# Three seams between the stages of a fused recurrence and two expert layers: rows, zero rows, weights and token blocks in another order

## The chip, the cores and the metric

The kernel runs on one core of a Trainium2 chip. The metric is the device time of one execution in microseconds (us); for the kernel before, it is the median of three runs.

## What is computed

A delta-rule attention feeds two mixture-of-experts layers. All arithmetic is in float32.

```python
# 4 batches x 8 heads, 768 tokens, head size 48
k_n = k / (norm(k) + 1e-6)
for t in range(S):
    y[t] = q[t] @ state
    state = state + beta[t] * outer(k_n[t], v[t] - k_n[t] @ state)
x = y as [3072 tokens, 384]
# first layer: 8 experts, F = 1024, one expert for each token (argmax of x @ w_gate)
out[mask] = gate_w[mask] * eom[mask, e] * (relu(x[mask] @ w1[e]) @ w2[e])
# second layer: 4 experts, F = 1024, every token in all of them
out += p[:, e] * (relu(x @ w1[e]) @ w2[e])
```

## The kernel before, in words

Five engines run their own written-out programs and meet at semaphores. A wait names a count; a DMA adds 16 when it has landed. There is no scheduler: the order in the source is the order on each engine.

**Attention.** The sequence is cut into NC = 12 chunks of 64 tokens. In chunk c TensorE does predict, solve, advance and read_out, and between them the products that prepare chunks c + 1 and c + 3 (level16, level32, gram, query) and the gate logits of chunk c - 1 (gates_turned L835, gates_product L844, gates_back). ScalarE (ACT) copies what they leave: gates_taken (L1168), left16_taken (L1150), values (L1145), x_taken (L1161), logits_turned, left32_taken (L1155). At the head of chunk 10 ACT calls first_expert_up (L1215 to L1218): it waits until the six pieces of w1 of expert 0 have landed, and casts them (the high part of a float32 that is split in two float32r parts). GpSimd (POOL) scatters the rows of each chunk by expert into the DRAM tensor x_rows (L583), whose 8 regions each end in up to 128 rows that tail_rows (L356 to L359) fills with zeros.

**Passes.** NPASS = 31 passes of 128 rows follow; each belongs to one expert, and every expert's last pass may be part zeros. SP loads the rows of pass s into the only buffer xs_in (L531) when pass s - 1 has taken its own. TensorE's `both(s)` is up(s) (18 matmuls), tokens_turned(s + 1) (3 transposes, L940), down(s - 1) (24 matmuls), hidden_turned(s) (8 transposes, L969). A product is three matmuls (high by high, high by low, low by high: L933 to L935). VectorE (DVE) does relus, turned, y_taken (L1688) and hidden (hTh L1680, hTl L1682). Weights of expert e + 1 are loaded and cast by ACT, and POOL makes their low part (L597). The keep_warm call (L929) multiplies ones 36 times between the attention and the first pass.

**Second layer.** The 3072 tokens are three blocks q = 0, 1, 2 of 8 tiles; 16 slices of 256 hidden units (v) each take three steps s, one for each block: up2 (33 matmuls in 7 sums, a scheme that forms [2x2] block products from sums of the operands), then down2 of the step before (8 tiles of 6 matmuls). The tokens of a block are first turned (turn(n), n = 8q + 0..7, 3 transposes, L997), copied by ACT (tokens_hi, L1306 to L1310), mixed by POOL (tokens_mixed, L646 to L652) and finished by DVE (tokens_lo L1751, mixed_lo L1756). Block 0 is turned during passes 22 to 25, blocks 1 and 2 at the end of the passes and inside the first steps. DVE also does summed (L1769), g_lo_taken (L1773), added (L1782) and once the gate values of all tokens (L1727 to L1744; shares_scaled is its second part, L1736 to L1744). The results leave by 24 indirect DMAs of POOL (L703), one for each tile.

The order on TensorE at the end of the passes is written out by hand:

```python
            up(NPASS - 1)
            down(NPASS - 2)
            hidden_turned(NPASS - 1)
            turn(QT)
            turn(QT + 1)
            down(NPASS - 1)
            turn(QT + 2)
            turn(QT + 3)
```

Here QT = 8. down(s) waits for hT_lo (DVE's hidden(s)) and for y_ok (DVE's y_taken(s - 2), which empties bank 4). turn(n) waits for x2T_read, which counts the tokens_lo that have emptied a bank.

## Time and profile before

| | us |
|---|---|
| median of 3 runs | 1475.72 (1472.4 to 1476.86) |
| the profiled execution, its own time | 1467.39 |
| its span, first to last instruction | 1465.5 |
| TensorE busy | 1393.4 (95%) |
| VectorE busy | 1030.3 (70%) |
| ScalarE busy | 344.8 (24%) |
| GpSimd busy | 375.8 (26%) |
| mean granted TensorE clock | 0.973 of full speed |

The 40 slices of the profile's page are 36.6 us each. TensorE is busy 9 tenths or more in nearly all slices from the fourth on; the exceptions are the slices at 293 to 366 us (8, 7), 366 to 403 us (8) and 659 to 696 us (7). In the same places the row of the granted clock leaves 9. The attention ends at about 350 us, the passes at about 664 us; the second layer takes the rest. The time of an execution is 1.9 us more than its span.

### The profile page before, as it was taken

How to read it: one execution, taken by the hardware profiler on the slowest of the kernel's cores; microseconds unless marked ns; L12 is line 12 of the kernel's file. 1: busy time of each engine (PE TensorE's matmuls, PEld its weight loads, DVE VectorE, ACT ScalarE, POOL GpSimd, SP SyncE). 2: the span in 40 equal slices, each digit the busy share in tenths (PEclk: the TensorE clock that was granted, in tenths of full speed). 3: DMA queues.
4: the chain of work that ended last, by engine and by line, in shares of the span. 5: the costliest groups of instructions: out<-in, count | busy, mean ns of one | idle time of the engine just before them, and what ended most of it. 6: DMA issues, size and time to landing. Idle time of an engine off the chain costs nothing.

```text
span 1465.5 us, 37247 instructions
## 1 busy us (share of the span) xinstructions
PE 1393.4 (95%) x14185; PEld 1277.8 (87%) x14186; DVE 1030.3 (70%) x1924; ACT 344.8 (24%) x810; POOL 375.8 (26%) x465
## 2 busy tenths in 40 slices
PE   5799999988899999997899999999999999999997
PEld 4789999977799999996899999999999999999996
DVE  5567777736566666667777777777777777777775
ACT  2345555431111111112211111111121111111111
POOL 1000101101444444337412121212212121212125
PEclk7999999989899999998999999999999999999999
DMA  6545554344433333010000000000000000000003
GB/s 132 112 98 105 126 107 116 83 121 141 142 108 109 109 109 109 18 39 22 11 12 21 11 21 11 22 11 21 11 22 20 12 21 11 21 11 21 11 11 119
DMA packets 101976, 85.67 MB, mean 58 GB/s; under 512 B 57520, under 2 KB 93488, under 8 KB 101872
## 3 DMA queue, kind: packets, MB, share of 16 engines
q1 hardware_dynamic: 83632, 49.32, 14.0%
q10 hardware_dynamic: 15168, 25.15, 5.3%
q0 software_dynamic: 3072, 9.71, 1.8%
q8 instruction: 77, 1.26, 0.4%
q14 instruction: 27, 0.22, 0.1%
HBM read 67.97 MB, written 16.18 MB: 57 GB/s over the span
## 4 chain that ended last, share of the span: by engine, by line
PE 89%; DMA 4%; DVE 3%; SPq 2%; issue 1%; ACT 1%; POOL 0%; ACTq 0%; POOLq 0%; DVEq 0%
PE bank L933 23%; PE bank L935 23%; PE bank L934 23%; PE bank L709 11%; PE bank L969 2%; PE bank L824 2%; PE bank L827 2%; PE bank L844 1%; ACT R L1123 1%; DMA kq_sb<-in_kq_dram 1%; PE bank L940 1%; SPq L449 1%; DMA inverse_blocks<-inverse 1%; DMA x_rows<-zeros 1%; PE bank L997 1%
## 5 line engine op out<-in xcount | busy, mean ns | idle before, releaser
L1784 DVE SCALAR_TENSOR_TENSOR y_all<-bank,aux_all,y_all 128x384 f32<-128x384 f32 x360 | 218.0, 616 | 102.3 <-PE bank L935 100.1
L1769 DVE TENSOR_TENSOR sums<-bank,sums 128x512 f32<-128x512 f32 x336 | 223.6, 688 | 60.0 <-PE bank L935 47.2
L933 PE MATMUL bank<-v2h,gTh 128*128 128x384 f32 x768 | 258.3, 336 | 3.0 <-DVE y_all L1782 2.3
L935 PE MATMUL bank<-v2h,gTl 128*128 128x384 f32 x768 | 257.7, 336 | 0.0
L934 PE MATMUL bank<-v2l,gTh 128*128 128x384 f32 x768 | 257.4, 335 | 0.0
L1322 ACT ACTIVATE gTh<-sums 128x512 fp32r<-128x512 f32 x192 | 110.9, 624 | 610.0 <-PE bank L935 608.0
L933 PEld LDWEIGHTS bank<-v2h,gTh 128*128 128x128 f32 x768 | 144.7, 188 | 5.8 <-DVE y_all L1782 2.7
L597 POOL TENSOR_TENSOR w_split_sb<-w_raw,w_split_sb 128x384 fp32r<-128x384 f32 (+1 forms) x98 | 107.0, 1142 | 165.6 <-ACT w_split_sb L1278 165.6
L934 PEld LDWEIGHTS bank<-v2l,gTh 128*128 128x128 f32 x768 | 144.7, 188 | 1.8
L1773 DVE SCALAR_TENSOR_TENSOR gTl<-sums,gTh 128x512 fp32r<-128x512 f32 x192 | 140.1, 770 | 7.3 <-ACT gTh L1322 4.3
L935 PEld LDWEIGHTS bank<-v2h,gTl 128*128 128x128 f32 x768 | 144.5, 188 | 0.0
L933 PE MATMUL bank<-w_split_sb,hTh 128*128 x248 | 86.5, 349 | 4.2 <-DVE hTl L1682 4.2
L682 POOL CAST v2h<-v_raw 128x384 fp32r<-128x384 f32 x32 | 15.3, 508 | 290.5 <-PE bank L935 290.5
L668 POOL CAST vA<-vA_raw 128x384 fp32r<-128x384 f32 (+1 forms) x48 | 24.3, 545 | 253.7 <-PE bank L935 253.6
L934 PE MATMUL bank<-w_split_sb,hTh 128*128 x248 | 84.1, 339 | 0.0
L935 PE MATMUL bank<-w_split_sb,hTl 128*128 x248 | 84.0, 339 | 0.0
L583 POOL DMA_INDIRECT x_rows<-rows_st,pos x24 | 26.3, 1097 | 215.9 <-PE bank L827 206.7
L933 PE MATMUL bank<-x_plain,vA 128*128 128x512 f32 x192 | 75.7, 394 | 6.2 <-DVE x_mixed L1756 6.2
L933 PE MATMUL bank<-w_split_sb,xsTh 128*128 (+1 forms) x186 | 76.9, 413 | 1.2 <-DVE xsTl L1664 1.2
L935 PE MATMUL bank<-x_plain,vA 128*128 128x512 f32 x192 | 76.4, 398 | 0.0
L934 PE MATMUL bank<-x_plain,vA 128*128 128x512 f32 x192 | 76.2, 397 | 0.0
L933 PE MATMUL bank<-x_mixed,vA 128*128 128x512 f32 x192 | 75.1, 391 | 0.0
(226 smaller groups left out, 2781.6 us busy)
## 6 DMA issues: line engine op xcount, KB each, us to landing
w_raw<-in_moe_w_dram ACTq DMA_DIRECT2D x14, 1536.0 KB, 7.1
xs_in<-x_rows SPq DMA_DIRECT2D x31, 203.0 KB, 2.4
v_raw<-in_moe_w_dram SPq DMA_DIRECT2D x15, 384.0 KB, 3.1
kq_sb<-in_kq_dram SPq DMA_DIRECT2D x28, 192.0 KB, 4.1
kt_sb<-in_kt_dram SPq DMA_DIRECT2D x24, 196.0 KB, 3.8
vt_sb<-in_vt_dram SPq DMA_DIRECT2D x24, 192.0 KB, 4.6
vA_raw<-in_moe_w_dram SPq DMA_DIRECT2D x15, 256.0 KB, 2.6
kq_sb<-in_kq_dram SPq DMA_DIRECT2D x14, 256.0 KB, 4.6
```

The costliest lines, as they stand in the source:

```text
L597: last = pool.tensor_tensor(lo[:, m, at_], raw[:, m, at_], hi[:, m, at_].bitcast(f32), ALU.subtract)
L709: return pe.matmul(dst, lhsT, rhs, start=True, stop=True)
L824: pe.matmul(bank[5 + p][half_rows(a), small(p, h)], kq_sb[half_rows(a), c % NKQ, 1, h], state[half_rows(a), c % 2, h], start=True, stop=False)
L827: last = pe.matmul(bank[5 + p][half_rows(a), small(p, h)], PT[half_rows(a), c % NPT, h], delta[half_rows(a), h], start=(c == 0), stop=True)
L933: pe.matmul(dst, lh, rh, start=first, stop=False)
L934: pe.matmul(dst, lh, rl, start=False, stop=False)
L935: return pe.matmul(dst, ll, rh, start=False, stop=last)
L969: ins = pe.transpose(bank[2 + half][:, 128 * m:128 * m + 128], h_sb[:, k0:k0 + 128], ident)
L1322: act.activation(sum_place(gTh, k), sums[:, SUM_TILE[k]], ACT.Relu).then_inc(g_hi, 1)
L1769: dve.tensor_tensor(out_, x, y, ALU.add).then_inc(sum_ok, 1)
L1773: dve.scalar_tensor_tensor(out=sum_place(gTl, k), in0=sums[:, SUM_TILE[k]], scalar=0.0, in1=sum_place(gTh, k).bitcast(f32), op0=ALU.max, o ...
L1784: dve.scalar_tensor_tensor(out=a, in0=src, scalar=share, in1=a, op0=ALU.mult, op1=ALU.add).then_inc(acc_ok, 1)
```

## The change

Seams one to three are the end of the attention, the first passes, and the way from the passes into the second layer; a fourth edit is at the end of the output.

1. **Weights of expert 0.** ACT's first_expert_up moves from the head of chunk 10 to behind values(11, 1) in that chunk.
2. **Rows and zero rows.** SP loads the rows of pass 1 (next_rows(1)) as soon as pass 0 has taken its own and the zero rows of expert 1 (second_zero) have landed, and only then issues the zero rows of experts 2, 4, 6. ACT issues the zero rows of expert 1 first, and those of 3, 5, 7 when the rows of pass 1 have landed (xs_load 32); its loads of the weights of expert 1 stand behind them. SP waits for all zero rows ahead of the rows of pass 2. Behind keep_warm 12 more products of ones, in float32r, are put.
3. **Last pass and token blocks.** The last pass has its own hTh_last, hTl_last, so that DVE's hidden(30) needn't wait for down(29). TensorE turns the first two tiles ahead of hidden_turned(30) and down(29), and spreads the other turns; down2(0) uses three banks, not two. On DVE hidden(30) comes first, y_taken(29) behind the first part of the gate values, shares_scaled behind four tokens_lo and a mixed_lo. The loads of vA and v2 and the cast of block 0's first tokens no longer wait for the last pass of expert 6; ACT does the cast of vA that POOL did. x_plain of blocks 0 and 1 change places in SBUF.
4. **Output.** POOL waits for two tiles at a time, but for the last two.

```diff
+        hTh_last = place("hTh_last", [128, KF, 128], f32r)
+        hTl_last = place("hTl_last", [128, KF, 128], f32r)
...
-        for q, (plain_at, mixed_at) in enumerate(((weights_base + 2 * w_size, weights_base),
-                                                  (common_end + 16384, weights_base + w_size),
+        for q, (plain_at, mixed_at) in enumerate(((common_end + 16384, weights_base),
+                                                  (weights_base + 2 * w_size, weights_base + w_size),
...
-            return bank[6 + n % 2 if n < 2 * QT else 3 + 2 * (n % 2) if n < 3 * QT - 2 else 5]
+            return bank[6 + n % 2 if n < 2 * QT else (3, 5, 0)[(n - 2 * QT) % 3]]
...
-               .then_inc(tail_zero if e else first_zero, 16)
+               .then_inc((first_zero, second_zero)[e] if e < 2 else tail_zero, 16)
...
+            sp.wait_ge(slots_ok, 1)
+            sp.wait_ge(second_zero, 16)
+
+            def next_rows(s):
+                sp.wait_ge(xsT_mm, s)
+                sp.wait_ge(aux_ok, s)
+                at_ = pass_i[0:1, 3, s:s + 1] if isinstance(s, int) else pass_i[0:1, 3, bass.ds(s, 1)]
+                row = sp.value_load(at_, min_val=0, max_val=NE * REG - 128)
+                load_rows(x_rows[bass.ds(row, 128), :])
+
+            next_rows(1)
             for e in range(2, NE, 2):
                 tail_rows(sp, e)
-            sp.wait_ge(slots_ok, 1)
-            sp.wait_ge(tail_zero, 16 * (NE - 1))
-            with sp.Fori(1, NPASS) as s:
-                sp.wait_ge(xsT_mm, s)
-                sp.wait_ge(aux_ok, s)
-                row = sp.value_load(pass_i[0:1, 3, bass.ds(s, 1)], min_val=0, max_val=NE * REG - 128)
-                load_rows(x_rows[bass.ds(row, 128), :])
+            sp.wait_ge(tail_zero, 16 * (NE - 2))
+            with sp.Fori(2, NPASS) as s:
+                next_rows(s)
...
+            up_weights_mixed(0)
             first_tokens()
-            up_weights(0)
             for j in range(BT):
                 tokens_mixed(j)
             down_weights(0)
             for j in range(BT, 2 * BT):
                 tokens_mixed(j)
             for v in range(1, NV):
-                up_weights(v)
+                up_weights_mixed(v)
+                up_weights_hi(v)
...
-                pool.wait_ge(acc_ok, QT * NQ * (NV - 1) + t + 1)
+                if t % 2 == 0 or t >= NT - 2:
+                    pool.wait_ge(acc_ok, QT * NQ * (NV - 1) + t + (2 if t < NT - 2 else 1))
...
+            for _ in range(12):
+                mul(bank[7][:, 0:128], ones_r[:], ones_r[:])
...
+                before = n - (1 if n < 2 * QT else 2)
                 if n >= 2:
-                    pe.wait_ge(x2T_read, n - 1)
+                    pe.wait_ge(x2T_read, before)
                 if n >= QT + 2:
-                    pe.wait_ge(x2T_raw, n - QT - 1)
+                    pe.wait_ge(x2T_raw, before - QT)
                 if n == 2 * QT:
                     pe.wait_ge(sum_ok, NSUM)
-                if n == 3 * QT - 1:
-                    pe.wait_ge(x2T_read, n)
-                    pe.wait_ge(x2T_raw, n - QT)
                 for m in range(KD):
...
-            down(NPASS - 2)
-            hidden_turned(NPASS - 1)
             turn(QT)
             turn(QT + 1)
-            down(NPASS - 1)
+            hidden_turned(NPASS - 1)
+            down(NPASS - 2)
             turn(QT + 2)
             turn(QT + 3)
+            down(NPASS - 1, hTh_last, hTl_last)
+            turn(QT + 4)
+            turn(QT + 5)
 
...
+                    elif isinstance(s, int) and s == 0:
+                        turned_here = (2 * QT + 5, 2 * QT + 6, 2 * QT + 7)[t]
+                        pe.wait_ge(x2T_read, turned_here + 1)
+                        pe.wait_ge(x2T_raw, turned_here + 1 - QT)
...
-            up2(0, 0, FIRST_BANKS, range(QT + 4, 2 * QT))
+            up2(0, 0, FIRST_BANKS, range(QT + 6, 2 * QT))
             pe.wait_ge(y_ok, NPASS + 1)
             tokens_ready(1)
             pe.wait_ge(sum_ok, NSUM)
-            up2(1, 1, UP_BANKS, range(2 * QT, 2 * QT + 6))
+            up2(1, 1, UP_BANKS, range(2 * QT, 3 * QT))
             pe.wait_ge(v2_ready, 1)
-            pe.wait_ge(x2T_read, 3 * QT - 2)
-            pe.wait_ge(x2T_raw, 2 * QT - 2)
-            down2(0, 0, DOWN_BANKS[0:2], range(2 * QT + 6, 3 * QT))
+            down2(0)
...
-                if c == NC - 2:
-                    first_expert_up()
...
                     values(c + 1, 1)
+                if c == NC - 2:
+                    first_expert_up()
                 if c >= 1:
                     logits_turned(c - 1)
                 x_taken(c, 1)
...
-            for e in range(1, NE, 2):
+            tail_rows(act, 1)
+            act.wait_ge(slots_ok, 1)
+            act.wait_ge(xs_load, 32)
+            for e in range(3, NE, 2):
                 tail_rows(act, e)
-            act.wait_ge(slots_ok, 1)
-            act.wait_ge(xs_load, 16)
             for e in range(1, NE):
...
-            act.wait_ge(y_mm, even_end)
             act.wait_ge(w_ready, NE)
             load_up(act, 0)
             load_down(act, 0)
             act.wait_ge(x2T_read, QT)
             act.copy(x_plain[0][:, 0], x_raw[:, 0].rearrange("p m t n -> p m (t n)")).then_inc(x0_hi, 1)
+            act.wait_ge(y_mm, even_end)
             act.copy(x_other[0][:, 0], x_raw[:, 1, 1:KD].rearrange("p m t n -> p m (t n)")).then_inc(x0_hi, 1)
+            act.wait_ge(vA_link, 3)
+            act.copy(vA[:, 0], vA_raw[:]).then_inc(vA_hi, 1)
             act.wait_ge(x0_mixed, 1)
             act.copy(x_mixed[0][:, 0], mixed_raw[0][:]).then_inc(x0_hi, 1)
             act.wait_ge(diff_ok, 1)
...
-            y_taken(NPASS - 2)
...
+            hidden(NPASS - 1, hTh_last, hTl_last)
...
-            hidden(NPASS - 1)
             tokens_lo(QT)
             tokens_lo(QT + 1)
-            shares_scaled()
-            y_taken(NPASS - 1)
+            y_taken(NPASS - 2)
             tokens_lo(QT + 2)
             tokens_lo(QT + 3)
             mixed_lo(0)
-            summed(0, FIRST_BANKS, 0)
+            shares_scaled()
+            y_taken(NPASS - 1)
             tokens_lo(QT + 4)
             tokens_lo(QT + 5)
-            summed(0, FIRST_BANKS, 1)
+            summed(0, FIRST_BANKS, 0)
             mixed_lo(1)
-            summed(0, FIRST_BANKS, 2)
             tokens_lo(QT + 6)
             tokens_lo(QT + 7)
-            for i in range(3, NSUM):
+            for i in range(1, 4):
                 summed(0, FIRST_BANKS, i)
             mixed_lo(2)
-            g_lo_taken(0, 0)
+            summed(0, FIRST_BANKS, 4)
+            summed(0, FIRST_BANKS, 5)
             mixed_lo(3)
-            for k in range(1, 4):
+            summed(0, FIRST_BANKS, 6)
+            for k in range(4):
                 g_lo_taken(0, k)
             summed(1, UP_BANKS, 0)
...
-            for i in range(4, NSUM):
-                summed(1, UP_BANKS, i)
+            summed(1, UP_BANKS, 4)
+            summed(1, UP_BANKS, 5)
+            tokens_lo(2 * QT + 6)
+            tokens_lo(2 * QT + 7)
             mixed_lo(5)
-            first = DOWN_BANKS[0:2]
-            added(0, 0, 0, 0, True, first)
-            added(0, 0, 0, 1, True, first)
-            tokens_lo(2 * QT + 6)
-            added(0, 0, 0, 2, True, first)
-            added(0, 0, 0, 3, True, first)
+            summed(1, UP_BANKS, 6)
+            for t in range(3):
+                added(0, 0, 0, t, True)
             mixed_lo(6)
+            added(0, 0, 0, 3, True)
             g_lo_taken(1, 0)
             g_lo_taken(1, 1)
-            added(0, 0, 0, 4, True, first)
-            tokens_lo(2 * QT + 7)
-            for t in range(5, QT):
-                added(0, 0, 0, t, True, first)
             mixed_lo(7)
+            for t in range(4, QT):
+                added(0, 0, 0, t, True)
             step(2, 1, 0, True)
```

**SP, between the rows of pass 0 and the loop of the passes.** DMA x_rows<-zeros is tail_rows, xs_in<-x_rows the load of a pass's rows. Before:

```order
L531 DMA xs_in<-x_rows 128x406 [waits scattered1,scattered0,scattered2,first_zero,front_zero]
L357 TENSOR_LOAD tail_i
L357 ISA x2
L358 ISA
L358 DMA x_rows<-zeros 128x406
...
L544 UNCONDITIONAL_BRANCH [waits tail_zero,slots_ok]
L547 ISA [waits aux_ok,xsT_mm]
```

(The four rows of tail_rows stand there three times.) And now:

```order
L534 DMA xs_in<-x_rows 128x406 [waits scattered1,scattered0,scattered2,first_zero,front_zero]
L550 TENSOR_LOAD pass_i [waits xsT_mm,aux_ok,second_zero,slots_ok]
L550 ISA x2
L534 ISA
L534 DMA xs_in<-x_rows 128x406
L360 TENSOR_LOAD tail_i
...
L557 UNCONDITIONAL_BRANCH [waits tail_zero]
```

The wait for all zero rows has moved from ahead of pass 1's rows to ahead of pass 2's.

**DVE, from the relus of the last pass on.** x_plain and x_other with a bank are tokens_lo, y_all<-y_all,bank is y_taken. Before:

```order
L1688 TENSOR_TENSOR y_all<-y_all,bank 128x384
L1727 TENSOR_REDUCE gate_tok<-aux_all 128x24 [waits aux_ok]
...
L1680 CAST hTh<-bank 128x512 [waits hT_mm,rchain]
L1682 TENSOR_TENSOR hTl<-bank,hTh 128x512 [waits hT_hi]
...
L1751 TENSOR_TENSOR x_plain_126<-bank,x_plain_126 128x3x128 [waits x2T_hi]
...
L1736 TENSOR_REDUCE gate_tok<-gate_small 128x24 [waits exp_ok]
...
L1744 TENSOR_TENSOR aux_all<-aux_all,gate_tok 128x24x4 [waits rchain]
```

And now:

```order
L1706 CAST hTh_last<-bank 128x512 [waits hT_mm]
L1708 TENSOR_TENSOR hTl_last<-bank,hTh_last 128x512 [waits hT_hi]
...
L1819 TENSOR_REDUCE gate_tok<-aux_all 128x24 [waits aux_ok]
...
L1765 TENSOR_TENSOR x_plain_128<-bank,x_plain_128 128x3x128 [waits x2T_hi,rchain]
...
L1714 TENSOR_TENSOR y_all<-y_all,bank 128x384
...
L1770 TENSOR_TENSOR x_mixed_125<-mixed_raw_127,x_mixed_125 128x4x128 [waits mix_hi]
L1750 TENSOR_REDUCE gate_tok<-gate_small 128x24 [waits exp_ok]
```

hidden(30) no longer stands behind y_taken(29) and the gate values, and y_taken(29), for which down(30) waits, now stands behind both.

**ACT, in chunk 10.** Now (before, the CAST of w_split_sb stood first, ahead of both rows of xT_gate):

```order
L1192 COPY xT_gate<-bank 128x3x128 [waits lt_mm,xt_mm]
L1192 COPY xT_gate<-bank 128x3x128
L1174 COPY Z_79<-bank 128x32x16 [waits z16_mm]
...
L1169 ACTIVATE vt_sb<-vt_sb,length 128x48 x8
L1242 CAST w_split_sb<-w_raw_106 128x3072 [waits s_mm,w1_in]
L1198 COPY logits_T<-bank 16x256 [waits lg_mm,lt_mm]
...
L1179 COPY Z_80<-bank 128x16x32 [waits z32_mm]
```

TensorE's read_out and level16_right wait for the first three of these, gates_back and level32_right for the last two.

## Rows read from the trace of the kernel before

**Rows 1.** Windows; the columns are stretch, length, busy by engine, clock, DMA.
```profile
core 0: us, PE busy (x) PEld busy (x) DVE busy (x) ACT busy (x) POOL busy (x), PEclk, DMA share, GB/s
310.35:313.33 2.98, 0.00 (x1) 0.03 (x1) 0.00 (x0) 2.98 (x3) 0.00 (x0) 0.76 0.28 99
313.33:325.60 12.27, 12.27 (x184) 10.26 (x186) 1.59 (x3) 5.17 (x20) 2.15 (x3) 0.50 0.34 99
663.65:689.77 26.12, 17.29 (x90) 15.12 (x89) 24.14 (x40) 7.38 (x21) 22.74 (x33) 0.89 0.05 16
689.77:716.73 26.96, 23.12 (x105) 19.75 (x106) 18.63 (x33) 9.15 (x23) 12.73 (x21) 0.85 0.05 15
735.00:1450.00 715.00, 714.29 (x3650) 654.62 (x3649) 553.40 (x857) 124.69 (x224) 168.73 (x229) 1.00 0.06 19
```

**Rows 2.** Chain in order of time (start, us, what), chunks 9 and 10.
```profile
290.86 1.85 PE bank L709 x61
...
316.98 3.39 PE bank L709 x64
...
328.74 5.89 PE bank L709 x192
```

**Rows 3.** Timeline of ACT, and the landings of the tile vt_sb.
```profile
310.05 2.75 ACT L1218 CAST w_split_sb<-w_raw 128x3072 fp32r<-128x3072 f32 x1 [10.96 <-DMA w_raw<-in_moe_w_dram]
...
DMA to landing us min/median/max: 2.9/3.5/4.0
```

**Rows 4.** Chain in order of time, first passes.
```profile
358.31 8.37 DMA x_rows<-zeros
...
367.79 3.56 DMA xs_in<-x_rows
...
379.52 0.33 PE bank L940 x3
384.01 0.87 PE bank L969 x8
...
393.58 0.87 PE bank L969 x8
```

**Rows 5.** Timeline of ACT's DMA issues and of POOL, first passes.
```profile
350.69 4.04 ACTq L358 DMA_DIRECT2D x_rows<-zeros  x4
...
369.31 15.22 POOL L597 TENSOR_TENSOR w_split_sb<-w_raw,w_split_sb 128x512 fp32r<-128x512 f32 x14 [17.63 <-ACT w_split_sb L1278]
```

**Rows 6.** Timeline of PE, what ended its idle time.
```profile
669.53 0.44 PE L933 MATMUL bank<-w_split_sb,hTh 128*128 x1 [4.19 <-DVE hTl L1682]
...
689.77 0.76 PE L933 MATMUL bank<-x_plain,vA 128*128 128x512 f32 x1 [4.64 <-DVE x_mixed L1756]
```

**Rows 7.** Chain in order of time: two turns, nine matmuls, two turns.
```profile
675.53 0.66 PE bank L997 x6
...
678.27 0.66 PE bank L997 x6
```

**Rows 8.** Timeline of DVE, end of the passes.
```profile
664.43 0.34 DVE L1727 TENSOR_REDUCE gate_tok<-aux_all 128x24 f32<-128x192 f32 x1
...
666.64 0.69 DVE L1680 CAST hTh<-bank 128x512 fp32r<-128x512 f32 x1
...
670.09 0.34 DVE L1736 TENSOR_REDUCE gate_tok<-gate_small 128x24 f32<-128x192 f32 x1
...
676.53 0.56 DVE L1688 TENSOR_TENSOR y_all<-y_all,bank 128x384 f32 x1 [0.79 <-DVE aux_all L1744]
...
688.03 1.48 DVE L1756 TENSOR_TENSOR x_mixed<-mixed_raw,x_mixed 128x512 fp32r<-128x512 f32 x1
```

**Rows 9.** Groups by line, 663.6 to 716.7 us: busy, mean ns.
```profile
L1756 DVE TENSOR_TENSOR x_mixed<-mixed_raw,x_mixed 128x512 fp32r<-128x512 f32 x8 | 7.0, 869 | 0.0
```

**Rows 10.** Timeline of POOL, output.
```profile
1440.49 0.97 POOL L703 DMA_INDIRECT out_dram<-y_all,id_i  x1 [4.66 <-DVE y_all L1784]
1441.76 0.97 POOL L703 DMA_INDIRECT out_dram<-y_all,id_i  x1 [0.30 <-issue]
```

105 lines of the change are left out of this document (56 added, 49 removed).

## The prediction

> **What bounds the kernel now.** I read the windows first, then the chain of waits in order of time, then each engine's timeline at the seams. In the second layer's steady stretch TensorE is busy 714.29 of 715.00 us at full clock, with VectorE busy 553 [rows 1]: nothing of the change is in that loop, and only matmuls could shorten it. The three seams look different. In 310.35 to 313.33 TensorE does nothing, and for the 12.27 us after it has a clock of 0.50, the 1.2 GHz level [rows 1]. Between the rows of pass 0 and of pass 1 the chain runs through DMAs and not through an engine [rows 4]. Of the 53.08 us from 663.65 to 716.73 TensorE is busy for 40.41, at a clock of 0.85 to 0.89, while VectorE is busy 24.14 of the first 26.12 us [rows 1]: there VectorE's order sets the end. All of these stretches are on the chain, so what is saved in them should reach the end, as long as the steady loop behind them stays full.
>
> **Seam one, weights of expert 0.** ACT stood 10.96 us in wait for the last piece of w1, then cast for 2.75 us, until 312.8 [rows 3]; the copies that read_out and level16_right wait for stood behind it. After the change they run at once: level16_left ends at 310.35, read_out(10, 0) follows (1.9 us, as in chunk 9), then level16_right (1.85 at full clock, rather than 3.39) [rows 2], gates_product (1.4), read_out (1.9) and level32_left (1.9), which ends at 319.3. ACT meanwhile waits for the values' second half, issued at 307.1, to land after 2.9 to 4.0 us [rows 3], so at 311.1; two groups of 8 activations (1.9 us each, an estimate from the time between chunk 9's copies) and a copy of 0.5 end at 315.4, the cast at 318.1, and three small copies at 319.9. So level32_right, which before ended where the row of 192 matmuls begins at 328.74 less its own 1.9, plus the predict in that row, starts at 320.0 rather than 328.7: **8.7 us less**. That is 3.0 us of idle time, about 5 of half clock, and the rest small waits. If the clock falls all the same, the 9 us of matmuls take nearer to 14 and only 4 are left. I take the upper end, since no idle time is left in front of them, and keep 4 for the range.
>
> **Seam two, rows and zero rows.** Before, the rows of pass 1 waited for zero rows that took 8.37 us to land beside the load of the weights of expert 1, and then took 3.56 us [rows 4]. Now they wait only for pass 0's own. The 12 extra products push tokens_turned(0) back; a transpose of the same size takes 0.11 (3 in 0.33) [rows 4], so 1.3 us. Pass 0's rows are then taken at 361.2, SP needs 1.1 us from a release to its issue (366.68 to 367.79) [rows 4], and 2.5 to 3.6 to land: 365.0. up(0) ends at 365.3 and up(1) at 371.6. But the wait is not gone. ACT issues the zero rows of experts 3, 5, 7 only now, 1.0 us each (4 in 4.04) [rows 5]: 366.1 to 369.1, landed at about 370.7, and the rows of pass 2 follow 1.1 + 3.6 us later, beside the weights: 375.5. TensorE turns them at 375.6 rather than 379.52 [rows 4], 3.9 less. It stood idle for 4 us ahead of that. Before, from the landing of pass 1's rows at 371.35 to 379.52 it took 8.2 us for work that at full clock, with 0.6 for VectorE, takes 0.33 + 0.87 + 4.2 + 0.6 = 6.0 [rows 4]; I charge the same 2.0 again behind the new gap. **1.9 less**, with bounds of 5 less (clock stays up) and 1 more. The weights of expert 1 are loaded 12 us later; POOL's 15.22 us on them [rows 5] then end at about 395, their first half at 387. Expert 1 begins with pass 4, whose up starts at 404.0, two passes of 9.57 after 384.88 [rows 4]; 1.9 less is 402. There are 15 us of cover.
>
> **Seam three, last pass and tokens.** The sizes: down is 24 matmuls between the end of the transposes at 379.85 and 384.01, 4.2; two turns 0.66; nine matmuls 678.27 - 676.19 = 2.1, so up2 with 33 is 7.6 [rows 4, 7]; down2 is 48 of the size of down's, 8.4. Before, down(30) waited 4.19 us for VectorE's hidden(30) [rows 6], which stood behind y_taken(29) and 2.2 us of gate values [rows 8]. Now hidden(30) starts at 660.4, the gate values end at 665.4, two tokens_lo at 666.8, y_taken(29) at 667.8 (its register load is 0.5 to 0.8). TensorE, after up(30) at 659.2, has turns 0.66, hidden_turned 1.0 and down(29) 4.2 until 665.0, then waits for VectorE twice and starts down(30) at 667.9, not 669.53: the wait has become a wait for y_ok. VectorE's next link is shares_scaled and y_taken(30), 677.09 - 670.09 = 7.0 us [rows 8], from 669.6 on, after two tokens_lo and a mixed_lo: 676.6. The third turn pair inside up2(0) waits for it, 2 us. Before, from the end of y_taken(30), 677.1, to the start of up2(1), 689.77, VectorE took 12.7 us. Of these, two tokens_lo and a mixed_lo (1.8) now stand ahead, and a g_lo of 1.4 behind; 9.5 are left, so up2(1) starts at 686.1, **3.7 less**. From there to up2(2) were 26.96 us [rows 1], in which TensorE's own work is 7.6 + 8 turns 2.6 + 8.4 = 18.6; the difference was 2.3 and 1.5 of idle time and about 4 of half clock. VectorE's own work there is 18.63 [rows 1]. With three banks and no half clock I expect 22.0: **4.9 less**, together 8.6.
>
> Row and rule differ on one thing here. At 716.73 TensorE had stood idle for 1.5 us and kept full clock; after 4.19 and 4.64 it fell to 1.2 GHz [rows 1, 6]. My new gaps are 1.4 to 2 us, so I let the clock stand. The Trainium skill, TensorE: Matmul & The Clock Gate, A second HAM failure mode: psum-queue depth-cycling, says that short idle times between groups, come often enough, make the clock swing too; the sum by it would lose the 4 us of half clock again. No row of this stretch shows that for gaps so short.
>
> **Output.** POOL starts a tile's DMA 1.27 us after the one before, of which 0.30 is idle whether it has a wait or not [rows 10], so fewer waits bring nothing. From 1440.49 on it runs behind without a pause to the end, and its start now waits for a second tile, 1.04 us later (6 matmuls of 0.174). **1.0 more**; bounds 0 and 1.3.
>
> **Sum.** -8.7 - 1.9 - 8.6 + 1.0 = -18.2. The profiled execution took 1467.39, of which 1465.5 is span; it would take 1449.2. The median of the runs is 8.3 us above it, and I carry the difference over as it is: 1475.7 - 18.2 = 1457.5. About 0.3% (4.4 us) is what a measurement of this kernel can tell from no change.
>
> **The rivals.**
> (a) *The clock falls at seam one as before.* For it: chunk 10's matmuls are small and the copies between them leave short gaps. Against: with the same gaps chunks 5 to 9 kept full clock. Seam one is then worth 4: 1462.2.
> (b) *VectorE is drawn out by POOL.* More of its work now lies beside POOL's. A mixed_lo took 0.87 us in the mean but 1.48 beside POOL's low part of v2 [rows 8, 9]; all eight at 1.48 make 4.9, and seam three gives 3.7: 1462.4. For it: POOL is busy 22.74 of 26.12 us there [rows 1]. The Trainium skill, SBUF — State Buffer, SBUF: two separate sides, says that an operation of VectorE with two inputs in SBUF and one of GpSimd lock each other out for a whole instruction; that speaks against putting more of them side by side. The trace agrees in kind (1.48), though most of the eight show less.
> (c) *More:* the clock stays up at seam two and down2 runs through: 4 to 8 less again, 1451.
> (d) *It doesn't do what it says.* ACT has the values' landing in place of w1's, SP has pass 2 in place of pass 1, down(30) has y_ok in place of hT_lo. If each new wait is as long as the old one, 1475.
> (e) *Slower: the weights of expert 1 are late.* They stand behind ACT's zero rows, and these behind the rows of pass 1. up(4) waits once w1's low part is later than 402, each us is a us, and the kernel is slower than before from 421 on, if a landing takes 34 us more than the 8 I allow. With 45: 1486. Nothing in the trace takes so long, hence the small chance.
>
> **How the numbers follow.** Forecast (1453 to 1461.5) 0.58; (a) 0.12; (b) 0.13; (c) 0.09; (d) 0.05; (e) 0.03. Predicted is the forecast's 1457.5. The range, 1449 to 1467, takes in (a), (b), their meeting, and (c). Faster by over 0.3%: 0.58 + 0.12 + 0.13 + 0.09 = 0.92; within 0.3%: 0.05; slower 0.03.
>
> **What would show it.** Seam one: no row of TensorE waiting for ACT's cast, and no stretch at 0.50 between 310 and 326. Seam two: the rows of pass 1 issued ahead of the zero rows of 2, 4, 6, up(1) some 7 us earlier, then a gap of about 4 us on the rows of pass 2. Seam three: down(30) behind a y_all of VectorE, up2(1) waiting under 2 us, no gap inside down2(0), and the span from up(30)'s end to up2(2) at about 49 us rather than 57.5. Output: 1 us more from TensorE's last matmul to the end. I am wrong if the clock row has as many stretches at 0.50 as before, if a gap of over 5 us opens at pass 2 or pass 4, or if the steady stretch is longer than 715 us for the same steps.

## The result and the profile after

The changed kernel takes 1458.3 us (median of 12 runs, 1452.37 to 1464.54), the kernel before 1475.12 (12 runs, 1464.19 to 1480.39). The ratio is 0.989, with a 95% interval of 0.987 to 0.992: about 16 us less. The forecast was 1457.5.

The profiled execution of the changed kernel took 1455.32 us with a span of 1453.4, 12.1 less than the 1465.5 of before. The sum of the prediction was 18.2. So the median came out as forecast, and the pair of profiles did not. Of the page, TensorE busy is 1392.4 (96%), VectorE 1026.1 (71%), and the mean granted clock 0.979 for 0.973. Its windows, where those of before are [rows 1]; the columns are stretch, length, busy by engine, clock, DMA:

```profile
284.53:300.84 16.31, 15.85 (x465) 14.60 (x465) 11.08 (x30) 7.35 (x25) 2.97 (x3) 1.00 0.41 129
300.84:307.82 6.98, 6.98 (x135) 6.92 (x131) 3.29 (x11) 0.00 (x0) 0.00 (x0) 0.51 0.43 88
307.82:322.39 14.57, 14.11 (x401) 12.87 (x401) 4.89 (x11) 9.33 (x25) 2.14 (x3) 1.00 0.52 158
322.39:329.74 7.35, 7.35 (x193) 7.30 (x193) 3.12 (x11) 0.04 (x1) 0.00 (x0) 0.77 0.10 30
656.90:682.04 25.14, 20.44 (x114) 17.78 (x113) 20.46 (x40) 7.37 (x21) 15.91 (x23) 1.00 0.02 5
682.04:703.48 21.44, 20.55 (x105) 18.33 (x106) 19.27 (x32) 8.02 (x21) 13.21 (x22) 0.92 0.06 19
735.00:1440.00 705.00, 704.29 (x3600) 645.62 (x3599) 544.57 (x845) 123.52 (x222) 169.98 (x231) 1.00 0.06 20
```

The reader is to see three things. At seam one the idle time is gone, but TensorE stands at the 1.2 GHz level for nearly 7 us from 300.84 on, where it had not in the profile before, and again for a part of 322.39 to 329.74. Taken together the time at that level is some 10 us here and was nearly 14 before (an estimate from the lengths and clocks of the windows, 12.27 us at 0.50 and a part of 2.98 at 0.76 in [rows 1]). Seam three is short and nearly all at full clock. The steady stretch is what it was: 0.71 us of 705 idle, as of 715.

The chain of waits, in order of time, at seams one and two; it answers to [rows 2] and [rows 4]:

```profile
298.93 8.90 PE bank L729 x192
...
314.60 1.85 PE bank L729 x64
...
322.39 7.35 PE bank L729 x192
...
355.43 2.81 DMA xs_in<-x_rows
...
361.33 3.03 DMA x_rows<-zeros
364.65 0.27 SPq L550
365.38 6.00 DMA xs_in<-x_rows
371.42 0.55 PE bank L962 x3
371.97 1.32 issue
...
395.54 0.67 issue
```

The row of 192 matmuls that had begun at 328.74 begins at 322.39, 6.35 earlier and not 8.7. The row of 192 ahead of it took 8.90 us for what takes 5.77 at full clock. The rows of pass 1 land at 358.24, without a wait for the zero rows. The next wait stands where it was expected, at the rows of pass 2, but the load took 6.00 us beside the weights of expert 1, and behind it TensorE stood for another 1.32 us put down to issue: the profile shows nothing that it waited for.

TensorE's timeline at seams two and three (start, length, idle time before it in brackets with what ended it), where those of before are [rows 6]:

```profile
362.32 0.79 PE L955 MATMUL bank<-w_split_sb,xsTh 128*128 x1 [1.85 <-issue]
371.42 0.55 PE L962 MATMUL bank<-const_sb,xs_in 128*128 128x128 f32 x3 [3.14 <-DMA xs_in<-x_rows]
...
665.50 0.44 PE L955 MATMUL bank<-w_split_sb,hTh_last 128*128 x1 [0.95 <-DVE y_all L1714]
...
673.34 0.94 PE L1017 MATMUL bank<-const_sb,y_all 128*128 128x128 f32 x6 [0.58 <-issue]
...
682.04 0.47 PE L955 MATMUL bank<-x_plain,vA 128*128 128x512 f32 x1 [2.29 <-DVE sums L1783]
...
702.32 0.44 PE L955 MATMUL bank<-v2h,gTh 128*128 128x384 f32 x1 [0.88 <-DVE y_all L1796]
```

down(30) waits 0.95 us for y_taken(29), as forecast, in place of 4.19 for hidden(30). up2(1) waits 2.29 in place of 4.64. The gap inside down2(0) is 0.88 in place of 2.33. At the output VectorE's last add ends at 1443.49 and GpSimd's last DMA starts at 1448.20, 4.71 later; before it was 1456.80 and 1460.26, 3.46 [rows 10].

To compare many profiles I cut the program at five events on TensorE that all kernels have. A: from gates_turned in chunk 9 to the first product of keep_warm. B: from there to tokens_turned(0). C: from there to tokens_turned(5). D: from there to tokens_turned(30). E: from the last product of up(30) to the start of up2(2). The starts come from the timeline of each profile; us:

| kernel (order at seam one, two, three) | A | B | C | D | E |
|---|---|---|---|---|---|
| before (old, old, old) | 64.32 | 9.75 | 49.94 | 241.78 | 57.56 |
| changed (new, new, new) | 58.85 | 9.41 | 52.77 | 241.78 | 46.80 |
| u_seam1 (old, new, new) | 61.05 | 11.05 | 53.37 | 249.56 | 45.81 |
| u_seam2 (new, old, new) | 60.18 | 9.41 | 56.58 | 241.78 | 46.73 |
| u_seam3 (new, new, old) | 60.53 | 10.91 | 52.80 | 251.84 | 58.58 |
| u_output (new, new, new) | 58.85 | 9.42 | 52.68 | 241.78 | 46.75 |
| again (new, new, new) | 59.36 | 9.42 | 52.69 | 241.78 | 46.72 |
| u_seam12 (old, old, new) | 64.49 | 10.84 | 56.16 | 241.78 | 46.80 |
| fill (new and products, new, new) | 60.51 | 11.04 | 51.93 | 259.92 | 46.66 |
| s3_buffer (new, new, new less a buffer) | 61.14 | 10.74 | 52.68 | 241.78 | 54.44 |
| rows_late (new, other, new) | 62.23 | 9.76 | 45.67 | 251.08 | 45.79 |
| rows_early (new, other, new) | 62.06 | 9.41 | 49.32 | 241.78 | 46.75 |
| two_rows (new, two buffers, new) | 57.99 | 10.84 | 42.43 | 241.77 | 46.95 |
| two_rows_less (new, two buffers, new) | 60.39 | 8.85 | 42.41 | 241.78 | 45.85 |

The experiments follow in the order in which they ran. The sets ran on different chips, on which the kernel before took 1480.4, 1500.0, 1495.5 and 1482.2 us, so kernels are compared by their ratio to it, or by the table.

### The profile page after: what moved, and what is told of

The parts are those of the page before. It is cut to its first block, busy times and chain, and to the rows that moved or that the text cites. A ratio compares the mean times of both kernels' runs of the same rounds, so it can differ in the third digit from the quotient of the medians.

```text
span 1453.4 us, 37267 instructions
## 1 busy us (share of the span) xinstructions
PE 1392.4 (96%) x14197; PEld 1278.0 (88%) x14198; DVE 1026.1 (71%) x1924; ACT 345.6 (24%) x811; POOL 374.8 (26%) x462
## 3 DMA queue, kind: packets, MB, share of 16 engines
q1 hardware_dynamic: 83632, 49.32, 13.9%
## 4 chain that ended last, share of the span: by engine, by line
PE 88%; DMA 3%; DVE 3%; issue 1%; ACT 1%; POOL 1%; SPq 1%; ACTq 0%; POOLq 0%; DVEq 0%
PE bank L955 23%; PE bank L957 23%; PE bank L956 23%; PE bank L729 12%; PE bank L991 2%; PE bank L844 2%; PE bank L847 1%; PE bank L864 1%; ACT R L1147 1%; POOL out_dram L723 1%; DMA kq_sb<-in_kq_dram 1%; PE bank L962 1%; DMA xs_in<-x_rows 1%; PE bank L855 1%; DMA inverse_blocks<-inverse 1%
## 5 line engine op out<-in xcount | busy, mean ns | idle before, releaser
L955 PE MATMUL bank<-w_split_sb,hTh 128*128 x240 | 84.5, 352 | 2.9 <-issue 2.9
L956 PE MATMUL bank<-w_split_sb,hTh 128*128 x240 | 81.8, 341 | 0.0
```

What stands on the lines that cost most here:

```text
L955: pe.matmul(dst, lh, rh, start=first, stop=False)
L956: pe.matmul(dst, lh, rl, start=False, stop=False)
```

## One seam put back at a time

**Seam one.** first_expert_up at the head of chunk 10 again:

```diff
+                if c == NC - 2:
+                    first_expert_up()
                 if ahead:
                     gram_scaled(c + 3, 0)
...
-                if c == NC - 2:
-                    first_expert_up()
```

> The changed kernel with seam one alone put back: ACT casts w1 of expert 0 at the head of chunk 10 again. By the prediction seam one is worth 8.7 us: 1458.3 + 8.7 = 1467.0, the idle stretch of about 3 us on TensorE returns at 310, and the row of 192 matmuls that level32_right opens, at 322.39 in the changed kernel, starts at about 328.7. The rival comes from the changed kernel's own trace: from the start of keep_warm in both only 4.8 us were gained, because TensorE's clock stood at 0.50 from 300 to 308.5 and from 324 to 328.5, where it had not before. If the new order brings those stretches, they are absent here, keep_warm starts at about 348.3 and the time is 1463.1. If they come by themselves in some executions, they can be absent or present here whatever the order, and the gain over many executions is nearer to 8 than to 4.8.

Ratio to before 0.9949 (0.9917 to 0.9981), 1470.9 us. The idle time on ACT's cast is back, though only 1.81 us of it, and the clock was at half before it came:

```profile
307.00:311.00 4.00, 4.00 (x98) 4.00 (x96) 1.24 (x2) 0.00 (x0) 0.00 (x0) 0.63 0.24 24
316.00:328.00 12.00, 10.19 (x206) 8.10 (x202) 2.16 (x5) 7.97 (x22) 1.95 (x2) 0.74 0.49 136
```

```profile
319.79 0.32 PE L844 MATMUL bank<-state,kq_sb 64*64 64x48 f32 x4 [1.81 <-ACT xT_gate L1192]
```

So the stretches at half clock don't belong to the new order. They come in both orders, at other places of chunks 9 to 11 in each profile. Column A tells what is left of the gain: the three profiles with the old order have 61.05, 64.32 and 64.49 (mean 63.3), the ten with the new one, without the kernel fill, 57.99 to 62.23 (mean 60.2). Seam one is worth 3.1 us in the mean, 5.5 in the pair of the result. The 3.1 is an indication and not more: only three profiles have the old order, and one of them, 61.05, lies among the new ones. The medians show no loss at all: on the same chip u_output, with the new order at seam one, took 1470.2, and the two intervals leave room for some 7 us either way.

**Seam two.** The order of rows and zero rows of before, with the 12 products:

```diff
-            next_rows(1)
             for e in range(2, NE, 2):
                 tail_rows(sp, e)
-            sp.wait_ge(tail_zero, 16 * (NE - 2))
-            with sp.Fori(2, NPASS) as s:
+            sp.wait_ge(slots_ok, 1)
+            sp.wait_ge(tail_zero, 16 * (NE - 1))
+            with sp.Fori(1, NPASS) as s:
...
-            tail_rows(act, 1)
-            act.wait_ge(slots_ok, 1)
-            act.wait_ge(xs_load, 32)
-            for e in range(3, NE, 2):
+            for e in range(1, NE, 2):
                 tail_rows(act, e)
+            act.wait_ge(slots_ok, 1)
+            act.wait_ge(xs_load, 16)
```

> The changed kernel with the order of rows and zero rows put back: pass 1's rows wait for all zero rows again, ACT writes its four zero rows together; the 12 products stay. By the prediction this order was worth 1.9 + 1.3 us (the products had cost 1.3): 1461.5, and TensorE stands idle for about 7 us ahead of pass 1. The rival is the reading of the two traces: from the start of keep_warm to hidden_turned of pass 3 it was 54.8 us before (348.34 to 403.14) and is 57.1 now (343.52 to 400.65), since TensorE now stops twice, for the rows of pass 1 and for those of pass 2, and drops to half clock twice. Then this kernel needs 1.0 less than the changed one in that stretch and takes 1457.3, or up to 2.3 less, 1456.0.

Ratio 0.9927 (0.9891 to 0.9962), 1468.7 us, the same as its neighbours within the intervals. TensorE's timeline:

```profile
376.25 0.90 PE L954 MATMUL bank<-const_sb,xs_in 128*128 128x128 f32 x3 [7.58 <-DMA xs_in<-x_rows]
396.67 0.55 PE L954 MATMUL bank<-const_sb,xs_in 128*128 128x128 f32 x3 [2.44 <-DMA xs_in<-x_rows]
398.52 0.44 PE L947 MATMUL bank<-w_split_sb,hTh 128*128 x1 [1.30 <-issue]
```

The stop of 7.6 us is there, as both readings had it. The second stop, at a later pass, was in neither, and the profile before does not have it. It is one load of rows, issued at 390.5, 0.91 us behind a load of weights, which took 6.17 us to land; u_seam12 below has the same at 402.0 (6.43 us). What such loads have in common is shown at rows_late. With it stretch C takes 56.58, 3.8 more than in the changed kernel; without it, in the profile before, 49.94, 2.8 less. So the old order takes the one or the other, and whether stretch C gains or loses by the new one depends on which is met. Both expectations missed.

**Seam three.** The kernel before with the other three edits, so that the orders at the end of the passes are the old ones on all engines; on TensorE, for one:

```diff
             up(NPASS - 1)
+            down(NPASS - 2)
+            hidden_turned(NPASS - 1)
             turn(QT)
             turn(QT + 1)
-            hidden_turned(NPASS - 1)
-            down(NPASS - 2)
```

> The kernel before with seams one, two and the output changed, seam three as it was. By the prediction seam three is worth 8.6 us: 1466.9, and from the end of the last up product to the start of up2(2) it takes 57.3 us. The traces read 46.6 for that in the changed kernel, so 10.7 less: 1469.0. The rival that more of VectorE's work beside GpSimd's draws it out has already fallen if this stretch is 57 here.

Ratio 1.003 (0.9998 to 1.0062), 1483.9 us: all of the measured gain is gone. Not all of it is seam three's by the profile, whose stretch D is 10.1 us longer as well. The nearer comparison is with u_output on the same chip: 13.7 us more, where E is 11.8 longer and the output's wait accounts for 1.3. Stretch E is 58.58, and its four stops are those of before:

```profile
682.37 0.68 PE L944 MATMUL bank<-w_split_sb,hTh 128*128 x1 [4.23 <-DVE hTl L1694]
703.46 0.76 PE L944 MATMUL bank<-x_plain,vA 128*128 128x512 f32 x1 [4.42 <-DVE x_mixed L1768]
725.22 0.44 PE L944 MATMUL bank<-v2h,gTh 128*128 128x384 f32 x1 [2.33 <-DVE y_all L1794]
730.55 0.47 PE L944 MATMUL bank<-x_plain,vA 128*128 128x512 f32 x1 [1.51 <-DVE x_mixed L1768]
```

In the eleven profiles that have seam three whole, E lies between 45.79 and 46.95. It is the steadiest number of the table.

**Output.** GpSimd waits for each tile:

```diff
-                if t % 2 == 0 or t >= NT - 2:
-                    pool.wait_ge(acc_ok, QT * NQ * (NV - 1) + t + (2 if t < NT - 2 else 1))
+                pool.wait_ge(acc_ok, QT * NQ * (NV - 1) + t + 1)
```

> The changed kernel with GpSimd's wait for each tile of the output again, and not for two. By the prediction 1.0 us less, 1457.3; from the last add of VectorE to the last output DMA 3.5 us (1456.80 to 1460.26 before) and not 4.7 (1443.49 to 1448.20). The rival is that fewer waits save GpSimd time in each tile: then it takes as long as the changed kernel or longer, and the pitch of the DMAs is over 1.28 us. Up to 1430 this kernel is the changed one instruction for instruction, so it shows besides whether the stretches at half clock at 300 and 324 us belong to the order or to the single execution.

Ratio 0.9942 (0.9906 to 0.9979), 1470.2 us. The end of GpSimd's timeline, with VectorE's last add ending at 1445.35:

```profile
1447.49 0.97 POOL L722 DMA_INDIRECT out_dram<-y_all,id_i  x1 [0.30 <-issue]
1448.77 0.97 POOL L722 DMA_INDIRECT out_dram<-y_all,id_i  x1 [0.30 <-issue]
```

From the last add to the last DMA are 3.42 us, and 4.71 in the changed kernel: the wait for two tiles costs 1.3. The pitch is 1.28 in both. The medians are too wide to show it: the ratio is 0.9942 here, and 0.9893 for the changed kernel in the set of the result. In windows of 1.5 us the stretches below full clock lay at 301.5 to 310.5 and 325.5 to 330, where the changed kernel has its own.

## Both first seams, the clock, and the rows of pass 2

**The changed kernel again**, with no edit, as a yardstick.

> The changed kernel itself, beside the others of this set, since the four kernels before it ran on a chip where the kernel before took 1480.4 us and not 1475.1. It gives the yardstick: with GpSimd's waits for each tile it took 1470.2 there, so I expect 1470 to 1472 if these runs meet the same spread. In its profile: from the gate transposes of chunk 8 to the start of keep_warm 58.9 to 60.5 us, as in the three profiles with ACT's new order; from tokens_turned(0) to tokens_turned(5) 52.7 to 53.4; from the last up product of pass 30 to up2(2) 46.7.

Ratio 0.992 (0.9868 to 0.9972), 1485.9 us, where 1470 to 1472 had been expected. Its stretches are as expected; most of what is longer on this chip lies before chunk 9, which begins at 301.84 and not at 284.53.

**Seams one and two both put back**, by the two edits of the kernels u_seam1 and u_seam2 together.

> The changed kernel with seams one and two both put back, so only seam three, the output and the 12 products are changed. By the prediction seams one and two were worth 8.7 + 1.9 + 1.3 = 11.9 us, and this takes 11.9 more than the changed kernel. By the runs so far (each seam put back alone left the time within 2 us of the kernel that lacks only the output's edit) nearly all of the gain is seam three's, and this is within 3 us of the changed kernel.

Ratio 0.9924 (0.988 to 0.9968), 1483.2 us: not told apart from the changed kernel, where 11.9 us more had been forecast. The parts of its one profile say otherwise: A is 5.1 longer than in the profile taken beside it, B and C together 4.9. With runs of the changed kernel that spread from 1471 to 1501 the two intervals leave room for about 10 us either way, so the medians neither confirm these 10 us nor exclude them; the 11.9 of the prediction is not borne out.

**More work for TensorE in chunks 9 and 10.** Three times in each:

```diff
+                if NC - 3 <= c <= NC - 2:
+                    pe.wait_ge(r_ok, 2 * NC)
+                    for _ in range(4):
+                        mul(bank[0][:, 256:384], ones_r[:], ones_r[:])
```

> The changed kernel with three times 4 products of ones (128x128, 0.11 us each at full clock) in each of the chunks 9 and 10: behind solve, behind level16_left and ahead of level32_right. One group of four lies in a gap of 0.46 us, the others cost 0.9 us in a chunk, 1.8 in all. The question is why TensorE's clock stands at 0.50 from 300 to 308.5 and from 324 to 328.5 in the changed kernel, with no idle time of more than 0.46 us before it: chunks 9 and 10 lack the gram and query products that the others have, and the products left are 64x64. If more work on TensorE keeps the clock up, the two stretches go, and with them 3.1 + 1.5 us less the 1.8: 2.8 us faster than the changed kernel. If the clock falls for another reason, the kernel is 1.8 us slower and the stretches stay.

Ratio 0.9946 (0.9907 to 0.9984), 1488.5 us. The profiled execution is the slowest of its twelve (1504.98 us), and its stretch D is 18.1 us longer, so it is read for chunks 9 and 10 alone. There the clock stayed up:

```profile
320.00:330.00 10.00, 9.02 (x223) 7.64 (x221) 3.66 (x6) 3.45 (x12) 1.77 (x3) 1.00 0.52 158
330.00:340.00 10.00, 9.67 (x285) 9.35 (x283) 6.55 (x19) 0.86 (x2) 0.00 (x0) 1.00 0.61 141
340.00:350.00 10.00, 9.00 (x227) 7.60 (x225) 1.59 (x3) 7.70 (x21) 2.15 (x3) 1.00 0.45 129
```

But A was 60.51, no less than its neighbours: the 24 products took more than their 2.6 us, since five gaps of 0.33 to 0.46 us, put down to the issue of instructions, came with them. One profile at full clock, among others with one or two stretches at half, does not show that the products kept it up. That stays open. No gain in time shows, in A or in the ratio.

**All zero rows early, the weights behind pass 2's rows.**

```diff
-            tail_rows(act, 1)
-            act.wait_ge(slots_ok, 1)
-            act.wait_ge(xs_load, 32)
-            for e in range(3, NE, 2):
+            for e in range(1, NE, 2):
                 tail_rows(act, e)
+            act.wait_ge(slots_ok, 1)
+            act.wait_ge(xs_load, 48)
```

On SP the zero rows of 2, 4, 6 stand ahead of next_rows(1) again, and second_zero alone is awaited there.

> The changed kernel, with all zero rows issued at once as before, expert 1's still counted apart, so that pass 1's rows wait for that one alone, and with ACT's loads of the weights of expert 1 held back until the rows of pass 2 have landed. Theory one: what TensorE waits for at pass 2 is the chain zero rows after the rows of pass 1 (3.03 us on ACT's queue and 3.0 to land) and then a load of 6.00 us beside the weights. Here nothing of this chain is left: the rows of pass 2 are issued as soon as those of pass 1 are taken and land in under 3 us, TensorE doesn't stop, and tokens_turned(0) to tokens_turned(5) takes 6.1 + 6.5 + 3 x 9.57 = 41 to 44 us and not 52.8, so the kernel is 8 to 11 us faster than the changed one. Theory two: the rows of 31 passes and the weights share the DMA engines, and a stop at pass 2 only moves to pass 4, since the weights of expert 1 now come 2 us later: then the five passes still take 50 or more and the kernel is within 2 us of the changed one.

Ratio 0.987 (0.9805 to 0.9936), 1480.3 us. C fell by 7 us to 45.67, so the chain of zero rows and late rows was the wait. But D rose by 9.3: five of the passes up to the twelfth are 1.3 to 3.2 us longer, with a stop as below. DMA issues and TensorE around one of them:

```profile
441.26 0.38 ACTq L1287 DMA_DIRECT2D w_raw<-in_moe_w_dram  x1
442.16 0.34 SPq L534 DMA_DIRECT2D xs_in<-x_rows  x1
...
448.42 0.55 PE L962 MATMUL bank<-const_sb,xs_in 128*128 128x128 f32 x3 [1.20 <-DMA xs_in<-x_rows]
450.25 0.44 PE L955 MATMUL bank<-w_split_sb,hTh 128*128 x1 [1.29 <-issue]
```

And the same two issues in the changed kernel, taken beside it:

```profile
446.18 0.34 SPq L534 DMA_DIRECT2D xs_in<-x_rows  x1
446.26 0.40 ACTq L1287 DMA_DIRECT2D w_raw<-in_moe_w_dram  x1
```

Here is the cause of the stops that come and go. Weights that go out 0.90 us ahead of a pass's rows delay them: the slowest landing of rows in rows_late was 6.2 us, and the buffer is free too late to bear that. Rows that go out 0.08 us ahead of the weights are not held up: between 400 and 660 us the median landing in the changed kernel is 2.4 and the slowest 3.3. All fourteen profiles bear this out. Of the loads of rows that went out less than 1 us behind a load of weights, 19 in all, every one took 5.96 to 7.21 us; of those that went out 0.06 to 0.09 us ahead of one, 55 in all, none took more than 3.22 (median 2.55). A us more or less in the weights' chain turns one into the other for several passes in a row. In stretch D, rows_late has three such late loads and is 9.3 us longer, u_seam1 two and 7.8, u_seam3 two and 10.1, fill five and 18.1: 3 to 5 us for each. None of these edits was meant for stretch D, so its length has to be read apart from what an edit was meant to do.

## Two buffers, and the buffer of seam three

**Two buffers for the rows**, the odd one at the place of hTh_last:

```diff
+        xs_odd = place("xs_odd", [128, RW])
+        xs_in = (xs_even, xs_odd)
...
+                    sp.wait_ge(xsT_mm, s - 1)
+                    sp.wait_ge(aux_ok, s - 1)
...
+            with sp.Fori(1, NPASS // 2) as t:
+                next_rows(t * 2, 0)
+                next_rows(t * 2 + 1, 1)
...
+            with pe.Fori(0, 10) as t:
+                both(t * 2 + 1, (), 0, t + 1)
+                both(t * 2 + 2, (), 1, t + 1)
```

> Two buffers for the rows of the passes (the odd one lies where hTh_last will be), so that the rows of pass s + 1 are loaded while pass s is taken; all zero rows issued at once, only expert 1's awaited ahead of pass 1's rows; the weights of expert 1 behind the rows of pass 2; GpSimd's output waits for each tile again. The loops over the passes are written out by twos. Theory one: every stop of TensorE in the passes (7.6 us or 6.1 + 3.1 ahead of passes 1 and 2, and the stops of 1.5 us with 1.3 us behind them that some profiles show each time a load of weights goes out just ahead of a pass's rows) is a load of rows that is issued one pass too late. Then tokens_turned(0) to tokens_turned(5) takes 5.4 + 5.4 + 3 x 9.57 = 40 to 42 us, no pass behind it is longer than 9.57 or 10.22, and the kernel is 11 us faster than the changed one in the passes and 1.2 at the output: about 12 us. Theory two: the longer loops bring stops of their own while instructions are fetched, or the zero rows and the rows of pass 1 land late beside each other: then less than half of that is left.

Three other edits go with it: all zero rows early, the weights of expert 1 behind the rows of pass 2, both as in rows_late, and GpSimd's wait for each tile as in u_output.

Ratio 0.9777 (0.9734 to 0.9821), 1463.6 us, where the kernel before took 1495.5. C is 42.43, 10.3 less than in the changed kernel, and no later pass stops. Of these 10.3, rows_late with one buffer had 7.1; the second buffer's own share of C is the other 3.2, and it gives nothing back in D. What is left in C is no longer a DMA:

```profile
377.75 0.50 PE L962 MATMUL bank<-w_split_sb,xsTh 128*128 128x512 f32 x1 [1.24 <-DVE xsTl L1703]
...
385.30 0.50 PE L962 MATMUL bank<-w_split_sb,xsTh 128*128 x1 [1.62 <-issue]
```

**The same early zero rows with one buffer, the weights behind pass 1's rows** (xs_load 32 for 48 in the edit of rows_late, and the output's waits as in u_output):

> As the kernel whose weights of expert 1 wait for the rows of pass 2 (there tokens_turned(0) to tokens_turned(5) took 45.7 us, but six of the passes after it were 1.3 to 3.2 us longer than 9.57), but with the weights issued behind the rows of pass 1, as in the changed kernel, and GpSimd's output waits for each tile. If those later stops come from the weights' later start, they are gone here, pass 2's rows land beside the weights (some 6 us, so a stop of at most 3 us) and the kernel is 4 to 6 us faster than the changed one. If they come and go by themselves, some stay.

Ratio 0.9871 (0.9817 to 0.9924), 1476.4 us. C is 49.32, 3.4 less than in the changed kernel, and D is 241.78, without stops: as the first reading had it, the later start of the weights in rows_late had brought them.

```profile
390.43 0.55 PE L961 MATMUL bank<-const_sb,xs_in 128*128 128x128 f32 x3 [1.78 <-DMA xs_in<-x_rows]
392.26 0.44 PE L954 MATMUL bank<-w_split_sb,hTh 128*128 x1 [1.29 <-issue]
```

**Seam three without hTh_last.**

```diff
+            dve.wait_ge(y_mm, NPASS)
+            hidden(NPASS - 1)
-            hidden(NPASS - 1, hTh_last, hTl_last)
```

> The changed kernel, but the last pass's inner rows in the common buffer again, so that VectorE's hidden(30) waits for down(29) to end, as it did before; all orders as changed. By the prediction's reading of seam three VectorE's chain sets the end: hidden(30) starts at the end of down(29), 663.7 in the changed kernel's own time, and not at 658.2, everything behind it on VectorE is 5.5 us later, down(30) too, and the stretch from the last up product to up2(2) takes 46.8 + 5.5 = 52.3 us. The rival: VectorE has idle time behind it (1.04 + 0.33 + 0.27 + 0.79 us of waits up to y_taken(30)) that takes up some of it, and the gate values could run while it waits only if they stood first, which they don't: then 3 to 4 us more, 50 to 51.

Ratio 0.9944 (0.9906 to 0.9981), 1485.7 us. E is 54.44, 7.6 more, above both expectations. VectorE waits for down(29), and TensorE in turn for the tokens:

```profile
679.44 0.69 DVE L1704 CAST hTh<-bank 128x512 fp32r<-128x512 f32 x1 [6.06 <-PE bank L955]
```

```profile
684.88 1.51 PE L1015 MATMUL bank<-const_sb,y_all 128*128 128x128 f32 x6 [5.48 <-DVE x_plain L1764]
```

down(30) starts 5.7 later after up(30), which is the expected delay; the other 1.9 us come behind it, where down(30) and the turns ran at half clock after the long gap (from its start to up2(0) 7.07 us, against 4.92). With the other edits in place the second buffer is worth 7.6 us, where all of seam three is 10.8. How the rest divides among the spread turns, the three banks and VectorE's order was not tried.

**Two buffers without the 12 products:**

```diff
-            for _ in range(12):
-                mul(bank[7][:, 0:128], ones_r[:], ones_r[:])
```

> The kernel with two buffers for the rows, without the 12 products of ones. The prediction charged these products 1.3 us. The profile of the changed kernel says less: the rows of pass 0 were issued at 349.67, and loads that meet nothing else land after 2.3 to 2.8 us, so at 352.2, while the products end at 352.8; without them TensorE would wait 0.7 us for the rows. So I expect 0.5 to 0.6 us less from the start of keep_warm to tokens_turned(0), 8.9 for 9.4, where the clock holds. The rival: it is for these products that the clock stays up in up(0), and without them a stretch at 0.50 behind tokens_turned(0) costs 1.5 to 3 us more. And the kernel with two buffers is measured a second time: a ratio to the kernel before of 0.978 within its interval, and 42 to 43 us for the first five passes.

Ratio 0.9758 (0.9722 to 0.9795), 1444.6 us, where the kernel before took 1482.2. B is 8.85: the products cost 0.6, and without them TensorE waits for the rows of pass 0 instead. No stretch at half clock follows tokens_turned(0):

```profile
363.46 0.55 PE L969 MATMUL bank<-const_sb,xs_even 128*128 128x128 f32 x3 [0.57 <-DMA xs_even<-x_rows]
```

This profile also shows what the second buffer does. Five of its loads of rows between 429 and 574 us went out 0.9 us behind a load of weights and took 5.96 to 6.40 us to land, as long as those behind which the kernels with one buffer stop. Here no pass is longer for them: D is 241.78.

The ratio of the changed kernel was 0.989 and 0.992, so both kernels with two buffers beat it clearly, by 17 to 24 us. By the table C (10.3) and the output (1.3) make 11.6 of these. Executions of the changed kernel with stops in D could be the rest, but no profile of it has caught one, so that is not shown. The intervals of the two kernels overlap, and no difference between them is shown but B's 0.6.

## Why the prediction was right, and where not

**Seam one, forecast 8.7, measured 5.5 in the pair of profiles and 3.1 over thirteen.** The step that failed is the clock: "I take the upper end, since no idle time is left in front of them". The order on ACT did what it should, and no row of TensorE waits for the cast; at full clock the row of 192 would have begun 6.35 + 3.1 = 9.5 us earlier. But TensorE fell to the 1.2 GHz level with nothing but a gap of 0.46 us before it. What made it fall is not shown. Rival (a), at 4, was right in kind: the clock fell all the same. The argument against it, that chunks 5 to 9 kept full clock with the same gaps, did not hold in later sets: of the 12 profiles after the first two, nine show one or more such stretches between 125 and 275 us. The Trainium skill, TensorE: Matmul & The Clock Gate, A second HAM failure mode: psum-queue depth-cycling, which the prediction set against the trace at seam three, says that frequent short idle times make the clock swing. The trace of chunk 9 does not bear it out: TensorE was idle for 0.46 us in all of the 16.31 us ahead of the 6.98 us at 0.51, and the kernel fill, with five gaps of 0.33 to 0.46 us in chunks 9 and 10, stood at 1.00.

**Seam two, forecast 1.9, measured a loss of 2.5 in the pair** (B and C: 59.69 before, 62.18 now), and a gain of about 1 over all profiles (old order 59.69, 65.99, 67.00; new order 62.1 to 64.4). The steps were right in kind: pass 1 free, the wait moved to pass 2, the weights of expert 1 in time. Mis-sized were the landing of the zero rows ahead of pass 2's rows (3.03, not 1.6), that of pass 2's rows (6.00, not 3.6), the stop of 1.32 behind it, and the stretches at half clock, two and not one. The step that failed outright is that the old order's cost can be read from one profile: it has a second stop in two of three. The 12 products were charged 1.3 and cost 0.6.

**Seam three, forecast 8.6, measured 10.8.** This carries the result. The waits are those forecast, in their order; the sizes came out in its favour. From the last product of up(30) down(30) was forecast 8.7 later and came 8.8 later; up2(1) was forecast 26.9 after it and came 25.4 after it; the step to up2(2) was forecast at 22.0 and took 21.4. The link of VectorE that was sized too long is shares_scaled with y_taken(30): 7.0 us were carried over from before, and it took 5.2.

```profile
666.88 0.34 DVE L1750 TENSOR_REDUCE gate_tok<-gate_small 128x24 f32<-128x192 f32 x1
...
671.54 0.56 DVE L1714 TENSOR_TENSOR y_all<-y_all,bank 128x384 f32 x1 [0.79 <-DVE aux_all L1758]
```

GpSimd did nothing from 668.5 to 673.0 there, and before it was at work on vA and the tokens until 675.6, through most of that link; four of VectorE's operations in it that took 0.48 to 0.79 us before took 0.18 to 0.27 now. That the one is the cause of the other was not tested by itself.

Two signs that were named did not come: up2(1) was to wait less than 2 us and waited 2.29, and down2(0) was to have no gap and has one of 0.88. And "I let the clock stand" failed: the clock fell behind the 2.29 us, and not behind 0.95, 0.58 and 0.88. Over all profiles this too is a matter of the execution. Eleven have this wait at 2.28 to 2.31 us; in eight the clock fell behind it and E is 46.66 or more, in three (u_seam1, rows_late, two_rows_less) it stood and E is 45.8. Rival (b) found nothing: E is 46.8, and 57.6 less its 3.7 would be 53.9.

**Output, forecast 1.0 more, measured 1.3 more.**

**The sum.** By the pair of profiles the terms are 5.5 - 2.5 + 10.8 - 1.3, with 0.5 less from the longer start: 12.0 of the span's 12.1. The medians lie 16.8 apart. The profile before was among its faster executions (1467.39 against 1475.12), and I carried that difference over as constant. It need not be: an old order that in most executions has 6 to 7 us of stops more in the first passes than the one I read would account for the rest. That fits u_seam2 and u_seam12, but it is argued; those executions of the kernel before were not seen. So 1457.5 against 1458.3 is in part two errors, seam one too high and seam two's old order too cheap, that took each other away. It is luck in a further way: the gain is not the same from set to set. The changed kernel again gained 12 us on 1500.0 (interval 4 to 20), and u_output, which should be the faster by 1.3, gained 8.6 on 1480.4 (3 to 14). The 18.2 of the sum lies near the end of the first interval and outside the second.

## What to carry to other kernels

A wait that is moved to the next load is safely gone only if that load has a buffer to go to: with the second row buffer the first passes lost 10.3 us and the later ones nothing, where no order of issuing with one buffer gave more than 7.1, and that one gave 9.3 back in later passes. Two DMA queues that start within a us of each other race; look which goes first in a good and a bad profile before giving either a price. And read an engine's stretch in several executions before you charge idle time and clock as one sum: where the clock also falls without a longer gap ahead of it, a filled gap may give back little more than itself: here 3.1 us in the mean, for gaps of 1.66 to 2.98.
